# Attention of the next batch and the dense stages of this one in common slots, with two PSUM banks for dense products and a DFT folded over channels

## What is computed

```
scores = q @ k.T / sqrt(64);  keep scores >= rowmax - tau;  attn = softmax;  x = attn @ v
xk = mu_k*x + (1-mu_k)*x_prev;  xr = mu_r*x + (1-mu_r)*x_prev      # x_prev: x one position back
x2 = sigmoid(xr @ w_r) * (relu(xk @ w_k)**2 @ w_v)                # 512 -> 1024 -> 512
u  = x2 + real(fft(fft(x2, axis=positions), axis=channels))
out = u + relu(layernorm(u) @ w_ch1) @ w_ch2                      # 512 -> 2048 -> 512
```

## Time and profile before

| | us |
|---|---|
| median of 3 runs | 1146.94 |
| lowest, highest | 1143.72, 1150.26 |
| the profiled execution | 1145.29 |
| its span in the trace | 1143.5 |
| busy: TensorE, VectorE, ScalarE, GpSimd | 1097.4, 716.5, 451.6, 397.8 |

### The profile page before, as it was taken

The page is one execution under the profiler, slowest core; times in us unless marked ns, Lnnn a source line. Parts: engine busy times, 40 slices in busy tenths (PEclk is TensorE's granted clock), DMA queues, the critical chain, the costliest instruction groups (busy, mean ns, idle before and its releaser), DMA issues.

```text
span 1143.5 us, 21451 instructions
## 1 busy us (share of the span) xinstructions
PE 1097.4 (96%) x7600; PEld 1067.1 (93%) x7600; DVE 716.5 (63%) x1466; ACT 451.6 (39%) x1004; POOL 397.8 (35%) x355
## 2 busy tenths in 40 slices
PE   5999999999999999999999999899999999999998
PEld 5889898999998899998899999799999999999998
DVE  6998984997974897985998887554131231323111
ACT  3776422677432677432677534231111111111110
POOL 4774573661352561351661333541211111110100
PEclk9999999999999999999999999899999999999999
DMA  8620020220020221020210202410101010010000
GB/s 244 205 65 4 1 68 20 87 67 23 2 85 2 88 56 35 1 59 28 86 45 2 93 1 71 170 60 19 37 1 56 1 56 0 0 55 0 28 1 28
DMA packets 29331, 55.76 MB, mean 49 GB/s; under 512 B 3376, under 2 KB 9648, under 8 KB 29232
## 3 DMA queue, kind: packets, MB, share of 16 engines
q1 hardware_dynamic: 29232, 54.46, 15.2%
HBM read 45.01 MB, written 9.44 MB: 48 GB/s over the span
## 4 chain that ended last, share of the span: by engine, by line
PE 79%; DVE 10%; issue 5%; POOL 3%; ACT 2%; DMA 1%; SPq 1%; DVEq 0%; POOLq 0%; ACTq 0%
PE PB L613 19%; PE PB L615 18%; PE PB L614 18%; PE PB L665 11%; PE PB L636 7%; PE PB L649 6%; DVE probs L1124 2%; POOL mix_l L518 1%; DVE neg_s L1103 1%; DVE gate L1243 1%; DVE k_sql L1253 1%; DVE k_sq L1250 1%; DVE mix_v L1171 1%; DVE mix_h L1180 1%; POOL u_sb L577 1%
## 5 line engine op out<-in xcount | busy, mean ns | idle before, releaser
L1330 DVE SCALAR_TENSOR_TENSOR h_lo<-PB,h_hi 128x384 fp32r<-128x384 f32 x96 | 53.4, 557 | 260.6 <-ACT h_hi L1052 260.6
L1052 ACT ACTIVATE h_hi<-PB 128x384 fp32r<-128x384 f32 x96 | 47.1, 491 | 339.9 <-PE PB L615 339.9
L665 PE MATMUL PB<-v_sb,probsT 128*128 128x64 f32 (+1 forms) x1440 | 177.9, 271 | 0.0
L665 PEld LDWEIGHTS PB<-v_sb,probsT 128*128 128x128 f32 x1440 | 172.8, 193 | 0.0
L1124 DVE SCALAR_TENSOR_TENSOR probs<-neg_s,thresh,exps 128x576 f32<-128x576 f32 x144 | 146.7, 1019 | 1.9 <-PE PB L649 1.8
L613 PE MATMUL PB<-un_h,w1h 128*128 128x384 f32 x384 | 134.2, 349 | 1.5 <-DVE un_l L1307 1.5
L885 ACT ACTIVATE exps<-neg_s,negmax 128x576 f32<-128x576 f32 x144 | 112.3, 780 | 55.2 <-DVE neg_s L1103 54.2
L614 PE MATMUL PB<-un_l,w1h 128*128 128x384 f32 x384 | 130.8, 341 | 0.0
L613 PE MATMUL PB<-h_hi,w2h 128*128 128x384 f32 x384 | 130.7, 340 | 0.0
L615 PE MATMUL PB<-un_h,w1l 128*128 128x384 f32 x384 | 130.3, 339 | 0.0
L615 PE MATMUL PB<-h_hi,w2l 128*128 128x384 f32 x384 | 129.5, 337 | 0.0
(11 more groups left out here) (139 smaller groups left out, 2518.6 us busy)
## 6 DMA issues: line engine op xcount, KB each, us to landing
q_raw<-qT_dram SPq DMA_DIRECT2D x64, 160.0 KB, 3.1
k_raw<-kT_dram SPq DMA_DIRECT2D x64, 144.0 KB, 3.1
w_raw<-w_dram SPq DMA_DIRECT2D x8, 1024.0 KB, 9.3
u_scr<-u_sb SPq DMA_DIRECT2D x4, 1152.0 KB, 4.8
u_in<-u_scr SPq DMA_DIRECT2D x6, 768.0 KB, 4.8
out_dram<-o_sb SPq DMA_DIRECT2D x24, 192.0 KB, 1.9
v_sb<-v_dram SPq DMA_DIRECT2D x4, 1024.0 KB, 5.6
wk_raw<-w_k_dram SPq DMA_DIRECT2D x1, 2048.0 KB, 14.2
```

The costliest lines, as they stand in the source:

```text
L665: last = nc.tensor.matmul(bank(6 + p)[:, i * DH:i * DH + width], probsT[:, j % 2, kt * P128:(kt + 1) * P128], v_sb[:, kt, cols], start=kt ...
L1330: nc.vector.scalar_tensor_tensor(h_lo[:, ft % 3, :], bank(4 + ft % 3)[:, 0:W], 0.0, h_hi[:, ft % 3, :].bitcast(F32), ALU.max, ALU.subtract ...
```

## The change

**One loop of slots.** Attention's 144 tiles are numbered through all batches. Every engine runs one loop over slots n; in slot n it does its step of tile n (or n-3, n-4 and so on, as before) and then what `run_beside` gives it: parts of the dense stages of batch d, each of which carries the slot, counted from the first tile of batch d+1, in which it is due. `Beside` is a generator that is advanced to that slot. On ScalarE the dense part stands between `exp(n)` and `copy_units(n-2)`. The dense stages of batch d so run beside the attention of batch d+1; those of the last batch run in the same order with no tile beside them. Loops over batches are gone; the text is written out for all four.

```diff
+X_AT = [3, 4, 5, 6]
+MIX_AT = [4, 5, 6, 7, 8, 9, 10, 11, 12, 13, 14, 15, 18, 19, 20, 21]
+Y_AT = [35, 35, 35, 36, 36, 36]
+U_AT = [37, 37, 38, 38, 38]
+FOLD_AT = [32, 34]
+V_ORDER = [(0, 1, 2, 3), (0, 3, 1, 2)]
+def k_at(c, i):
+    return 10 + (c * 240 + 48 + i * 12) * 25 // 480
+        def run_beside(stages, n):
+            for d in range(B):
+                for stage in stages[d]:
+                    stage.through(n - (d + 1) * TILES_BATCH)
```

```diff
-        def scores(j):
-            return PB[j % 2][:, :].rearrange("p (a n) -> p a n", a=2)[:, :, 0:HALF]
+        def scores(n):
+            both = PB[n % 2] if n < TILES_BATCH else PB[0]
+            return both[:, :].rearrange("p (a n) -> p a n", a=2)[:, :, 0:HALF]
+        def ring(i):
+            return bank(2 + i % 2)
+                    if n >= TILES_BATCH:
+                        pe.wait_ge(max_ready, n)
```

**Who does what.** ScalarE rounds the mixed values (`mix_h`), GpSimd takes the low part of the square (`k_sql`) and all low parts of the fold. gate+1 and reciprocal stand beside the first four w_k products. For chunk 0 of the MLP GpSimd's sum of squares stands between the low parts of squares 6 and 7, and VectorE's inverse root, newton and scaling ahead of the first y_l:

```diff
+                            nc.gpsimd.tensor_tensor(k_sql[:, ft, :], k_sq[:, ft, :], k_sqh[:, ft, :].bitcast(F32), ALU.subtract).then_inc(ksql_ready, 1)
+                            if last and c == 1 and ft == 6:
+                                sum_squares(0)
```

**DFT folded over channels.** Channels are laid out so that tile t and tile 3-t mirror each other. `fold(d, t)` first adds and subtracts the two tiles over all 576 positions, then folds positions; channel 256, which has no partner, is folded alone on one row (`middle`) and enters as two matmuls of one row. The DFT over channels then has 2 x 3 matmuls per group instead of 4 x 3:

```diff
+                        for t in range(2):
+                            last = three(o, fold_h[kind][:, t, ss], fold_l[kind][:, t, ss], cd[:, 0, t, cols].bitcast(F32R), cd[:, 1, t, cols].bitcast(F32R), t == 0, kind == 1 and t == 1)
+                        if kind == 0:
+                            pe.wait_ge(foldl_ready, d * 5 + 5)
+                            nc.tensor.matmul(o, mid_h[0:1, ss], odd[0:1, :].bitcast(F32R), start=False, stop=False)
+                            last = nc.tensor.matmul(o, mid_l[0:1, ss], odd[0:1, :].bitcast(F32R), start=False, stop=True)
```

1298 lines of the change are left out of this document (655 added, 643 removed).

## The result

The changed kernel takes 1196.72 us (median of 4 runs, 1187.68 to 1202.76) against 1148.6 of before in the same comparison: a ratio of 1.0414, 95% interval 1.0334 to 1.0495. The forecast was 1176, the range 1138 to 1204. The direction and the range held, but the result lies outside the 1160 to 1190 that had the chance of 0.46, between (e)'s 1196 and (c)'s 1201. 20 us of the 48 were not in the forecast's sum, and most of what follows is about where they come from.

The account below looks back on a forecast made before the run. TensorE, busy 96% of the span, was taken as the bound. Start 17.2 + four batches' work 647 + first-batch waits 10 + shared 3 x 17 + last 33 + MLP 414 = 1172 span, forecast 1176 us, range 1138 to 1204.

Parts of the forecast that it names:

- (e): Rival: DFT tables, loaded anew for each batch, come late, 5 us each, 20 in all, 1196 us; chance 0.04.
- (c): Rival: each TensorE wait above about 3 us costs 1.7 us more through a lower clock, 25 us, 1201; chance 0.15.
- MLP, 414: MLP after the batches: sums' wait and lower clock there go, first matmuls start earlier, 423.3 down to 414 us.
- First batch, 10 of waits: First batch's attention: waits for rounding w_r and w_k stay, table splits move under it; 10 of 21 us, bounds 4 and 21.
- A shared batch, 17: TensorE's waits in each batch sharing slots: gates 7, lean slots 5, DFT 4.3, eighth mixed tile 0.7; 17 us together.
- Gates, 7: Slots 12 to 14 and 25 to 27: VectorE's reciprocals delay row maxima, 3.5 us each half, 7 a batch; bounds 0 and 9.
- Lean slots, 5: Slots 4 to 9 and 19, mixing with little product: serial chain 3.2 us against TensorE's 2.19; 5 a batch, bounds 0 and 8.
- DFT, 4.3: DFT of a batch: fold's last low part 2.1, two-bank ring 0.7, second DFT's fifth group 1.5; 4.3 us, bounds 2 and 8.
- Last batch, 33: Last batch's dense part, nothing beside it: waits of 30 us plus 3 for restarts, 33; bounds 20 and 45.
- (a): Rival: holes do get filled, shared batches wait only 5 us for their DFT, the last 20; reported 1127; chance 0.15.
- (b): Rival: gain and loss cancel, shared batches wait 10 us, the last 26; reported 1148; chance 0.12.
- (d): Rival: GpSimd's low parts block VectorE's port, some 40 of 64 at 0.4 us each, 16 us, 1192; chance 0.08.

Follow-up runs that it names:

- e9: e8 with gate+1 and reciprocal one to a slot, the second DFT's fifth group in the fourth's bank, and GpSimd's splits in other slots: 1139.9 us.
- e1: The changed kernel run again without any edit: 1192.8 us, ratio 1.0399 to the kernel before.
- e7: Changed kernel with last-batch normalization, Newton step and scaling later, the middle row before the second fold, and later table splits: 1169.0 us.
- e3: Changed kernel with gate+1 and reciprocal spread one to a slot, behind the slot's squares: 1195.8 us.
- e12: e9 with gate+1 and reciprocal put back beside the square, as in the changed kernel: 1145.1 us, ratio 0.996 to the kernel before.
- e4: Changed kernel with the one-row operations of channel 256 behind the first fold, not the second, on three engines: 1181.3 us.
- e11: Changed kernel with the fifth group of the second DFT in the bank of the fourth, not the third: 1182.8 us.
- e8: e7 with idle matmuls, whose result nobody reads, ahead of TensorE's waits in the last batch: 1161.3 us, ratio 1.0088 to the kernel before.
- e10: Changed kernel without sharing, each batch's dense stages in one piece with its slot order and two banks: 1237.6 us, ratio 1.0778 to the kernel before.
- e5: Changed kernel with 22 idle matmuls a batch ahead of the wait for the fold's second low part: 1185.2 us.

## Why the prediction held, and where its sum did not

*Start and TensorE's own work.* 17.2 and 161.8 a batch. The start was 16.5. e9, at full speed throughout, has periods of 171.5 and 173.5 with 8.4 and 6.5 us of waits, so 165 of work a batch: 3 more than the sum had.

*MLP, 414.* 415.8, and 415.5 in e1. The wait for GpSimd's sums is gone, as said.

*First batch, 10 of waits.* The window to tile 36 is 94.8 us, for 78.8 + 2.1 + 10 = 90.9 in the sum. Later table splits in e7 gave nothing (95.2). In e9, with all of GpSimd's splits in new places, it is 91.5, but there the clock is 1.00 for 0.95, worth up to 5 us, so what the places give is not shown.

*A shared batch, 17.* The period was forecast at 178.8 and is 178.5 and 182.0. The parts are another matter: TensorE waits 10.7 and 10.5 us in the two, not 17. **Gates, 7:** the row maxima behind gate slots are waited for, as forecast, but for 1.6 us in each half (at 160.1 and 225.4 us in the first shared batch), 3.1 together, and not for 3.5 in each; the longest wait of a shared batch is the 1.8 us for mid_l and not, as put down, one for a row maximum. Second half of the first shared batch, VectorE, then TensorE:

```profile
219.62 0.30 DVE L1235 TENSOR_SCALAR gate<-gate 128x288 f32<-128x288 f32 x1
...
220.35 1.94 DVE L1244 RECIPROCAL gate<-gate 128x288 f32<-128x288 f32 x1
222.22 0.25 DVE L1235 TENSOR_SCALAR gate<-gate 128x288 f32<-128x288 f32 x1
...
222.74 1.95 DVE L1244 RECIPROCAL gate<-gate 128x288 f32<-128x288 f32 x1
224.60 0.69 DVE L1123 TENSOR_SCALAR_CACHE_REDUCE neg_s<-PB 128x576 f32<-128x576 f32 x1
```

```profile
223.52 0.29 PE L642 MATMUL PB<-mix_h,wkl 128*128 128x288 f32 x1
225.36 0.54 PE L662 MATMUL PB<-k_hi,q_hl 128*128 128x288 f32 x2 [1.55 <-DVE neg_s L1123]
```

A gate takes 2.4 to 2.6 us from one to the next, for 2.93 summed: gate+1 takes 0.25 to 0.30 where the earlier trace rows had 0.49 as a mean, and the operations overlap a little. And what the wait lasts is not what it costs: taken away in e3 it gives 6.4 us of waits in three batches, and in e9 against e12 1.2 us a batch by the windows. The step that failed is the reckoning through slots 25 to 27. **Lean slots, 5:** the transposes of tiles 36, 39 and 40 start at

```profile
111.28 0.71 PE L675 MATMUL PB<-ident,probs 128*128 128x128 f32 x5
...
120.72 0.71 PE L675 MATMUL PB<-ident,probs 128*128 128x128 f32 x5
124.25 0.71 PE L675 MATMUL PB<-ident,probs 128*128 128x128 f32 x5
```

Starts 3.0 and 3.5 us apart, near the forecast (3.2). But TensorE hardly waits here, its own work takes the time; the waits are 0.3, 0.5, 1.25 and 0.8 us in the four slots from 122 to 134 us, 2.9 for the forecast's 5. **DFT, 4.3:** the chain of the fold came out within 0.2 us, its waits within 0.5, and the price did not:

```profile
256.76 0.42 PE L662 MATMUL PB<-k_hi,q_hl 128*128 128x288 f32 x2
...
262.42 0.39 PE L640 MATMUL PB<-cd,fold_h 128*128 128x258 f32 x1 [0.75 <-POOL fold_l L562]
...
264.86 0.38 PE L809 MATMUL PB<-odd,mid_h 1*128 1x258 f32 x1 [1.81 <-POOL mid_l L565]
...
285.85 0.61 PE L640 MATMUL PB<-cs,y_h 128*128 128x290 f32 x1 [1.36 <-DVE summ L1282]
```

TensorE gets the last low part 8.1 us behind the last product (I said 8.3). The three waits are 3.9 us (I said 4.3, with 0.7 for the ring of two banks, for which TensorE did not wait). But the window around the last of them has a clock of 0.85 in e1, and e4 and e11, which take the second and the third away, win 11.5 and 10.0 us by the medians (6.3 and 5.6 between the profiles), where these waits last 6.6 and the fall by 0.9 four times comes to 3.4. The term had the waits and no clock.

*Last batch, 33.* Read as 110 us from the last tile to the MLP, it was 135.3, and 130.3 in e1. Its single waits were sized well: k_sql 4.2 (5 forecast), y_l 6.4 (4), the fold 3.6 and 1.1 (5), later banks 4.1 (5); all waits there are 25.6 us, for a sum of 30. "3 for restarts" is the term that failed. At a mean clock of 0.80 up to 135.3 x 0.20 = 27 us are the clock's; e8's idle matmuls, which shorten no chain, give 7.7 back by the medians, and e9 needs 109.4.

*The two-bank order* was priced only through its waits, 17 a batch. e10 gives its size apart: 26 us more of dense stage in the first period. Less the 19 that sharing wins there, this leaves the 7 by which the shared period exceeds 171.6; that is the same subtraction read twice, and no check on the forecast.

*Rivals.* (a) and (b) fell: the holes do get filled, but new ones open. (c) was the one nearest to the truth and had the wrong condition. I let the clock fall only behind waits of 3 us and gave it 25 us. In the shared batches it fell behind waits of 0.75 to 1.8 us following one another, which the earlier trace rows could not show, and it took up to 45 us more than before. Another row of the trace of before already spoke against the 3 us: the MLP's first matmul waits 1.5 us, and the window from 720.25 to 724.00 has a clock of 0.55.

```profile
720.25 0.69 PE L613 MATMUL PB<-un_h,w1h 128*128 128x384 f32 x1 [1.53 <-DVE un_l L1307]
```

(d), the blocked port: the masks' mean of 1012 ns is no higher than the 1019 of the earlier trace rows, but that of the squares is 638 ns for 486, 2.4 us more a batch on VectorE, and one case of it, below, stands ahead of a wait of TensorE's. The waits of 10 to 11 us leave no 5 us a batch for it. It was not tried alone. (e) fell: the larger table lands in 7.6 us, and no wait of any size ends with a transfer. The masks' and the squares' groups, and the table's row:

```profile
L1143 DVE SCALAR_TENSOR_TENSOR probs<-neg_s,thresh,exps 128x576 f32<-128x576 f32 x144 | 145.7, 1012 | 4.1 <-PE PB L675 2.5
...
L1241 DVE TENSOR_TENSOR k_sq<-k_relu 128x288 f32<-128x288 f32 x64 | 40.4, 638 | 26.8 <-ACT k_relu L994 26.6
...
cs<-cs_scr SPq DMA_DIRECT2D x4, 1740.0 KB, 7.6
```

So the forecast's periods were right by luck. Its waits were some 6.5 us a batch too dear (10.5 to 10.7 for 17), gates and lean slots above all. Against that stand 3 us of work a batch that the sum did not have, and a clock term that it did not have either: at most 3.6 us in the first shared period (0.98) and 7.3 in the second (0.96). Behind the last tile nothing made up for the missing term, where up to 27 us went to the clock, and from there come most of the 20 us by which the total was short.

## What to carry to other kernels

Price a wait of TensorE by what follows it: where waits of one or two microseconds come in a row, the matmuls behind them may run at half speed, and shortening four waits by 0.9 us each gave 10 us back by the medians and 5.6 between two profiles, and a move of the gates worth 4 to 5 us gave nothing while slow stretches were left. Compare span times (1 - clock) of the two kernels first; if that is the difference, look at the order in the places where the clock falls and not at the busiest engine. Before work is shared between stages, measure the dense stage that the shared order needs, run apart: a buffer less, an order by slots and a chain one link longer together cost more here than sharing gave.

## What the runs showed of the hardware

The clock was the surprise. In e1's first shared batch TensorE is at full speed up to the fold and at half speed behind its two waits of 0.75 and 1.81 us; the third window lies wholly in the slow stretch:

```profile
258.00:262.00 4.00, 3.27 (x28) 3.06 (x27) 3.98 (x12) 2.25 (x6) 0.76 (x2) 1.00 0.92 351
262.00:266.00 4.00, 2.17 (x11) 1.82 (x12) 1.38 (x6) 1.57 (x4) 3.75 (x5) 0.90 0.85 208
266.00:270.00 4.00, 4.00 (x18) 3.53 (x17) 1.25 (x3) 0.77 (x2) 3.56 (x3) 0.50 0.02 8
```

22 matmuls in that gap keep the clock at 1.00 in e5's first shared period. The Trainium skill, "TensorE: Matmul & The Clock Gate", section "A second HAM failure mode: psum-queue depth-cycling", describes a kernel whose short idle moments between groups of matmuls, as its PSUM banks rotate, make the clock swing between its two levels. The traces here agree, with waits of 0.75 to 1.8 us and a clock of 0.96. But e9 has waits of up to 1.9 us in its first shared period and no slow stretch before its last 4 us, so the length of a wait alone doesn't decide, and which sequence of them does stays open. Open as well is why two executions of one program, with the same waits, get 0.954 and 0.964.

GpSimd and VectorE can hold each other up: two squares of 0.45 us each took 3.23 while GpSimd took the low parts of k and q:

```profile
170.70 3.23 DVE L1241 TENSOR_TENSOR k_sq<-k_relu 128x288 f32<-128x288 f32 x2
```

```profile
169.95 1.94 POOL L499 TENSOR_TENSOR k_lo<-k_raw,k_hi 128x576 fp32r<-128x576 f32 x1
171.97 1.64 POOL L507 TENSOR_TENSOR q_hl<-q_raw,q_hl 64x640 fp32r<-64x640 f32 x1
```

Each square ends about 0.3 us behind one of GpSimd's operations (172.2 and 173.9, for 171.9 and 173.6). This agrees with the rule on the shared port pair that the prediction names. The next scores did not wait for it. But the low part of this second square, which GpSimd could make only from 175.3 to 176.6 us, is what TensorE waits for next; how much of that is the blocking, no run shows.

```profile
176.68 0.40 PE L640 MATMUL PB<-k_sqh,wvh 128*128 128x288 f32 x1 [0.57 <-POOL k_sql L555]
```
